# A retention layer and two expert layers in one kernel: decay tables made on TensorE, states as half blocks, first loads in another order

## The chip, the cores and the metric

One core of one Trainium2 chip runs the whole program. The metric is the device time of one execution in microseconds; the kernel before has a median of 1234.87 us over 3 runs (1234.5 to 1235.02).

## The reference

All arrays are float32. Retention is attention without a softmax: the score of query i and key j of head h is scaled and multiplied by gamma_h to the power i - j, and is zero for j > i. Two feed-forward layers follow on 4608 tokens of width 512.

```
gamma = 1.0 - 2.0 ** (-5.0 - arange(8))            # q, k, v: 8 x 8 heads x 576 x 64
ret = (q @ k.T / 8) * where(rel >= 0, gamma ** rel, 0)
x = ret @ v                                        # as 4608 x 512
h = max(x @ w1, x @ w2, x @ w3); x = h @ w_out     # 512 -> 768 -> 512
out = ((x @ u1) * (x @ u2)) @ u3 @ u_out           # 512 -> 1024 -> 1024 -> 512
```

## The kernel before, in words

**Two parts.** The first, 17 steps in the loop over m up to STEPS, computes the retention, two pairs of heads per step; there are 32 pairs n (a batch and two heads each). The second is a loop over 126 units of the dense products in four stages B, C, I, O. u3 and u_out follow each other with nothing between, so the first part also folds them into one matrix, in quarters of an eighth (wc_quarter). Every dense product is made from a high and a low fp32r part, so weights and tokens are split: ScalarE casts the high part, VectorE or GpSimd subtracts it for the low part.

**Retention in chunks.** A pair has 576 positions, which are 4 chunks of 128 and a tail of 64. Within a chunk TensorE makes scores (scores, L1000 and L1005), VectorE multiplies them by a table dec of powers of gamma (decay_scores L850, decay_tail L858), and TensorE multiplies by the values (values, L1048). Between chunks a state is carried: TensorE sums keys times decayed values (sum_state, L1021), VectorE scales the last state and adds (make_state, L872 and L875), and TensorE multiplies states by decayed queries (query_state, L1037). The two heads of a pair are 64 partitions each, so most matmuls use half of the array: rows or columns. query_state alone uses the whole array, on a 128 x 128 state with zeros outside the two diagonal blocks:

```
ps[:, bank, cols] += state[:, c - 1, :].T @ qdec[:, c - 1, :]
```

ScalarE decays the values (decay_values, L705, a factor per partition from vtab), reads results x (read_values, L716 and L721) and copies the folded block out (read_wc, L738); GpSimd decays the queries (decay_queries) with the table qtab. Where GpSimd works, the profile shows the helper's line, L589.

**What sets the order.** Each engine's program is written out by hand and waits on counting semaphores. Within step m TensorE makes the scores of pairs 2m and 2m + 1, then the quarters of that step, then query_state of the last step's pairs, sum_state of this step's, and values of the last step's. Quarters begin with step 3 (WC_FROM), two a step. The scores of pair n wait until x of pair n - 3 is read out (x_out), since they share a bank. All transfers are issued by SP in the order of its program: first the loads of pairs 0 to 3 with the tables between them, then step by step u3T and u_out blocks, keys for the next step, queries and keys (qk) for the step after it, stores of x, and values. The keys have two buffers; the queries four, the values six. A wait in SP's program holds all issues behind it.

## Time and profile before

| | |
|---|---|
| median of 3 runs | 1234.87 us |
| the profiled execution's own time | 1234.69 us |
| its span | 1232.9 us |
| TensorE matmul busy | 1216.6 us, 99% |
| VectorE, ScalarE, GpSimd busy | 761.3, 486.4, 433.7 us |
| transfers | 169.96 MB, mean 138 GB/s |

PE is TensorE (PEld its weight loads), DVE VectorE, ACT ScalarE, POOL GpSimd, SPq the issues of SP. A float32 matmul leaves two records. Times of a timeline count from the span's start. The first part ends near 177 us.

### The profile page before, as it was taken

Reading aid. Unit: us, or ns where it says so; the run is one execution under the profiler, and the core shown is the slowest. Engines: PE = TensorE matmul, PEld = TensorE weight load, DVE = VectorE, ACT = ScalarE, POOL = GpSimd, SP = SyncE. Lnnn points to the kernel's source line nnn. Section 1 sums busy time; section 2 is a strip of 40 time slices with the busy share of each in tenths; the row PEclk is TensorE's granted clock in tenths of the full one; section 3 lists DMA queues with packets and bytes.
Section 4 is the critical chain, followed back from the end, with each engine's and each line's share of the span. In section 5 each row is a group of like instructions: output and inputs, shape, how many; then the busy total and the mean of one; then the engine's idle time right before and its main releaser. Section 6 shows DMA issues by size and latency. Waiting matters only on the chain. (4 is left out here: it accounts for less than half of the span.)

```text
span 1232.9 us, 21160 instructions
## 1 busy us (share of the span) xinstructions
PE 1216.6 (99%) x8288; PEld 1202.2 (98%) x8288; DVE 761.3 (62%) x1192; ACT 486.4 (39%) x779; POOL 433.7 (35%) x234
## 2 busy tenths in 40 slices
PE   6999999999999999999999999999999999999999
PEld 5999999999999999999999999999999999999998
DVE  5666957844546364658876777453535366776553
ACT  3433544523223232326555544242323234554441
POOL 2644628220100102052967761202020217366550
PEclk9999999999999999999999999999999999999999
DMA  9999944120202112053455441213131343444441
GB/s 332 322 335 352 337 144 163 46 84 33 96 27 88 41 52 77 27 173 127 170 208 195 156 154 59 103 52 109 52 116 52 110 165 109 154 154 161 156 159 65
DMA packets 88084, 169.96 MB, mean 138 GB/s; under 512 B 9904, under 2 KB 59184, under 8 KB 87984
## 3 DMA queue, kind: packets, MB, share of 16 engines
q1 hardware_dynamic: 87984, 168.60, 39.3%
q8 instruction: 66, 1.08, 0.4%
q14 instruction: 34, 0.28, 0.1%
HBM read 106.70 MB, written 61.87 MB: 137 GB/s over the span
## 5 line engine op out<-in xcount | busy, mean ns | idle before, releaser
L1100 PE MATMUL ps<-chi,whi 128*128 128x384 f32 x2016 | 674.2, 334 | 2.1 <-ACT w L831 1.1
L1102 PE MATMUL ps<-chi,wlo 128*128 128x384 f32 x2016 | 673.5, 334 | 0.0
L1101 PE MATMUL ps<-clo,whi 128*128 128x384 f32 x2016 | 673.5, 334 | 0.0
L589 POOL TENSOR_TENSOR raw<-raw,raw 128x768 f32<-128x768 f32 (+3 forms) x102 | 267.1, 2640 | 588.8 <-DMA raw<-xd 203.6
L1100 PEld LDWEIGHTS ps<-chi,whi 128*128 128x128 f32 x2016 | 378.4, 188 | 4.2 <-ACT w L831 1.8
L1101 PEld LDWEIGHTS ps<-clo,whi 128*128 128x128 f32 x2016 | 378.5, 188 | 0.0
L1102 PEld LDWEIGHTS ps<-chi,wlo 128*128 128x128 f32 x2016 | 378.5, 188 | 0.0
L840 DVE TENSOR_TENSOR clo<-raw,chi 128x768 fp32r<-128x768 f32 (+2 forms) x168 | 252.4, 1530 | 31.8 <-ACT chi L763 31.8
L763 ACT CAST chi<-raw 128x768 fp32r<-128x768 f32 (+2 forms) x168 | 180.4, 1081 | 85.4 <-PE ps L1102 53.4
L831 ACT COPY w<-ps 128x384 f32<-128x384 f32 x126 | 60.6, 481 | 240.7 <-PE ps L1102 239.2
L818 ACT COPY u<-ps 128x384 f32<-128x384 f32 x126 | 60.7, 481 | 160.6 <-PE ps L1102 158.9
L956 DVE TENSOR_TENSOR h<-ps,u 128x384 f32<-128x384 f32 x66 | 36.6, 555 | 123.4 <-PE ps L1102 123.4
L930 DVE TENSOR_TENSOR h<-ps,w 128x384 f32<-128x384 f32 x66 | 36.6, 555 | 100.3 <-PE ps L1102 96.8
L930 DVE TENSOR_TENSOR w<-ps,w 128x384 f32<-128x384 f32 x60 | 33.4, 556 | 86.8 <-PE ps L1102 86.6
L797 ACT COPY s<-ps 128x384 f32<-128x384 f32 x126 | 60.5, 481 | 56.7 <-PE ps L1102 56.6
L810 ACT COPY h<-ps 128x384 f32<-128x384 f32 x66 | 31.6, 479 | 86.6 <-PE ps L1102 84.5
L956 DVE TENSOR_TENSOR u<-ps,u 128x384 f32<-128x384 f32 x60 | 33.2, 554 | 51.1 <-PE ps L1102 51.1
L840 DVE TENSOR_TENSOR wlo<-wraw,whi 128x768 fp32r<-128x768 f32 (+4 forms) x42 | 61.8, 1482 | 2.5 <-POOL wraw L589 2.3
L589 POOL TENSOR_TENSOR qdec<-qks,qtab 128x512 f32<-128x512 f32 x32 | 42.2, 1339 | 50.6 <-PE ps L1037 36.7
L589 POOL TENSOR_TENSOR wraw<-w,wraw 128x256 f32<-128x256 f32 (+2 forms) x21 | 24.7, 1177 | 92.2 <-DMA w<-wC 66.0
L589 POOL TENSOR_TENSOR wraw<-wraw 128x256 f32<-128x256 f32 (+2 forms) x42 | 47.4, 1130 | 1.6
L746 ACT CAST whi<-wraw 128x768 fp32r<-128x768 f32 (+4 forms) x42 | 43.9, 1054 | 5.0 <-POOL wraw L589 5.0
(43 smaller groups left out, 829.9 us busy)
## 6 DMA issues: line engine op xcount, KB each, us to landing
...
```

What stands on the lines that cost most here:

```text
L589: return nc.gpsimd.tensor_tensor(out_, a, b, op)
L746: nc.scalar.copy(whi[wi][:, s, :, :], wraw[wi][:, s, :, :]).then_inc(w_hi, 1)
L763: nc.scalar.copy(chi[st][pos][:, :, :], raw_block(tau, pos)[:, :, :]).then_inc(c_hi, 1)
L797: nc.scalar.copy(sbuf_s[it % 2][:, :], ps[:, X[it % 2], 0:N]).then_inc(s_made, 1)
L818: nc.scalar.copy(sbuf_u[it % 2][:, :], ps[:, X[it % 2], 0:N]).then_inc(u_made, 1)
L831: nc.scalar.copy(sbuf_w[it % 2][:, :], ps[:, X[it % 2], 0:N]).then_inc(w_made, 1)
L840: return nc.vector.tensor_tensor(out_, whole, hi.bitcast(f32), ALU.subtract)
L930: nc.vector.tensor_tensor(to[:, :], ps[:, Z[g % 2], 0:N], sbuf_w[g % 2][:, :], ALU.add).then_inc(sum22, 1)
L956: nc.vector.tensor_tensor(to[:, :], ps[:, Z[g % 2], 0:N], sbuf_u[g % 2][:, :], ALU.add).then_inc(sum12, 1)
L1100: nc.tensor.matmul(to, w1, x1, start=(start and k == 0), stop=False, skip_group_check=True)
L1101: nc.tensor.matmul(to, w1, x2, start=False, stop=False, skip_group_check=True)
L1102: last = nc.tensor.matmul(to, w2, x1, start=False, stop=(k == KH[st] - 1), skip_group_check=True)
```

## The change

Four things change.

1. The tables dec and qtab are no longer loaded. A small table of powers (pows, 8 partitions, one per head) is loaded, and TensorE makes the tables as outer products of powers by key and powers by query; VectorE masks the result to dec and ScalarE copies qtab. The value factors, a factor per partition for the states and the mask come in one other small load, cols. Fourteen matmuls on zeros (run_idle) stand between the first real ones.
2. A state is 128 x 64: each head has its block on its own partitions, and make_state works on both heads in one instruction with a factor per partition. query_state has two matmuls of 64 x 64 for each of before.
3. Loads: first keys and queries of pair 0 behind the two small tables; keys 0 to 3 have buffers of their own; the tails of the values are loaded apart, for two pairs at once, and so are the values from pair 4 on. Up to step 3 keys stand ahead of u3T and u_out. One of the u_out blocks is split on VectorE.
4. Quarters: step 3 has one of its two, step 4 has three, two of them at the step's end. Blocks of the stages C and O are loaded with a wait for each block.

```diff
 def quarters(m):
+    if m == WC_FROM:
+        return range(1)
+    if m == WC_FROM + 1:
+        return range(1, 2)
     if m >= STEPS - 2:
         return range(QUARTERS - 4 * (STEPS - m), QUARTERS - 4 * (STEPS - m) + 4)
     return range(2 * (m - WC_FROM), 2 * (m - WC_FROM) + 2) if m >= WC_FROM else ()
 
 
+def late_quarters(m):
+    return range(2, 4) if m == WC_FROM + 1 else ()
+
+
+
 
 U3_LOAD = {min(2 * kb + WC_FROM - 2, STEPS - 3): kb for kb in range(FT2)}
 U3_SPLIT = {min(2 * kb + WC_FROM - 1, STEPS - 2): kb for kb in range(FT2)}
-UO_LOAD = {1: (0, 1), 2: (2, 3)}
-UO_SPLIT = {2: (0, 1), 3: (2, 3)}
+UO_SPLIT = {2: (0,), 3: (1,), 4: (2, 3)}
...
+        dec = at("dec", [P, 2, 2, 2, CH], f32, o); o += HEADS * CH * 4
+        qtab = at("qtab", [P, PAIRS * CH], f32, o); o += PAIRS * CH * 4
+        cols = at("cols", [P, HEADS + PAIRS + CH], f32, o); o += (HEADS + PAIRS + CH + 4) * 4
+        vtab, gtab = cols[:, 0:HEADS], cols[:, HEADS:HEADS + PAIRS]
+        mask = cols[:, HEADS + PAIRS:]
+        pows = at("pows", [HEADS, 3 * P + PAIRS * CH], f32, 21504)
         vdec = [at(f"vdec{i}", [P, NC, P], f32, o + i * NC * P * 4) for i in range(2)]
...
+            def load_two_v(m):
+                n = 2 * m
                 if n >= 6:
-                    sp.wait_ge(valued, n - 5)
-                sp.dma_start(vs[n % 6][:, 0:NC * CH], vv[n, :, :]).then_inc(v_loaded[n % 6], 16)
-                sp.dma_start(vs[n % 6][TAIL:P, NC * CH:], vt[n, :, :]).then_inc(v_loaded[n % 6], 16)
+                    sp.wait_ge(valued, n - 4)
+                sp.dma_start(vs[:, n % 6:n % 6 + 2, 0:NC * CH], vv[n:n + 2, :, :].rearrange("n p c -> p n c")
+                             ).then_inc(v_loaded[v_sem(n)], 16)
+
+            def load_tails(m):
+                n = 2 * m
+                sp.dma_start(vs[TAIL:P, n % 6:n % 6 + 2, NC * CH:], vt[n:n + 2, :, :].rearrange("n p c -> p n c")
+                             ).then_inc(vt_loaded[m % 3], 16)
 
             def load_k(n):
-                if n >= 2:
+                if n >= 4:
                     sp.wait_ge(state_summed, n - 1)
-                sp.dma_start(ks[n % 2][:, :], kk[n, :, :]).then_inc(k_loaded[n % 2], 16)
+                sp.dma_start(keys_of(n)[:, :], kk[n, :, :]).then_inc(k_loaded[n % 4], 16)
...
-                for pos in (0, 3, 6, 2):
-                    if pos != 6 or t == 0 or st != O:
-                        load_raw_block(tau, pos)
-
-            def load_raw_rest(tau):
-                sp.wait_ge(c_lo, 7 * tau)
-                load_raw_block(tau, 6)
-
-            def load_decay(i, heads):
-                sp.dma_start(dec[:, heads, :], decay[:, heads, :]).then_inc(dec_loaded[i], 16)
-
+                for pos in blocks:
+                    if t and st in (C, O):
+                        if pos != 6 or st == O:
+                            sp.wait_ge(c_lo, 7 * (tau - 1) + pos + 1)
+                    load_raw_block(tau, pos)
+
+            sp.dma_start(pows[:, :], powers).then_inc(pows_loaded, 16)
+            sp.dma_start(cols[:, :], columns).then_inc(cols_loaded, 16)
             load_qk(0)
-            load_decay(0, slice(0, 2))
-            sp.dma_start(vtab[:, :], vdecay).then_inc(vtab_loaded, 16)
             load_v(0)
             load_k(0)
             load_qk(1)
-            load_decay(1, slice(2, 4))
             load_v(1)
             load_k(1)
             load_qk(2)
-            sp.dma_start(qtab[:, :, :], qdecay).then_inc(qtab_loaded, 16)
             load_qk(3)
-            load_decay(2, slice(4, HEADS))
             load_v(2)
             load_v(3)
+            load_k(2)
+            load_k(3)
+            load_tails(0)
             for m in range(STEPS):
+                if 0 < m < 4:
+                    for n in made_in(m + 1):
+                        load_k(n)
+                if m == 2:
+                    load_uo(1)
                 if m in U3_LOAD:
                     load_u3(U3_LOAD[m])
-                for i in UO_LOAD.get(m, ()):
-                    load_uo(i)
+                if m == 1:
+                    load_uo(0)
                 if m in P1_W_LOAD:
                     load_weight(P1_W_LOAD[m])
-                for n in made_in(m + 1):
-                    load_k(n)
+                if m >= 4:
+                    for n in made_in(m + 1):
+                        load_k(n)
                 for n in made_in(m + 2):
                     load_qk(n)
+                if m == 2:
+                    load_uo(2)
+                    load_uo(3)
                 for n in read_in(m):
                     if n >= PAIRS:
                         store_x(n)
-                for n in made_in(m + 2):
-                    load_v(n)
+                if m == 0:
+                    load_tails(1)
+                if 2 * m + 4 < NP:
+                    load_two_v(m + 2)
+                    load_tails(m + 2)
...
             for m in range(STEPS - 1):
+                for i in UO_SPLIT.get(m, ()) if m == 4 else ():
+                    split_uo(i)
                 if m in U3_SPLIT:
                     split_u3(U3_SPLIT[m])
-                for i in UO_SPLIT.get(m, ()):
-                    split_uo(i)
                 for n in made_in(m):
                     decay_queries(n)
+                for i in UO_SPLIT.get(m, ()) if m == 3 else ():
+                    split_uo(i)
...
-            for n in made_in(0):
-                decay_values(n)
+            act.wait_ge(idle_zeroed, 1)
+            nc.scalar.copy(idle[:, CH + 1:CH + 2], idle[:, CH:CH + 1])
+            decay_values(0)
+            act.wait_ge(qtab_powers, 1)
+            nc.scalar.copy(qtab[:, :], ps[:, S_WC, :]).then_inc(qtab_made, 1)
+            decay_values(1)
             for m in range(STEPS):
-                if m in U3_SPLIT:
+                if m == 2:
                     split_u3(U3_SPLIT[m])
                 for i in UO_SPLIT.get(m, ()):
                     split_uo(i)
+                if m in U3_SPLIT and m != 2:
+                    split_u3(U3_SPLIT[m])
                 if m in WC_READ:
                     read_wc(WC_READ[m])
                 for n in read_in(m):
...
             def make_state(n):
                 p = n % PAIRS
                 bank = S_WC if n == 1 else S_STATE
                 dve.wait_ge(state_summed, n + 2 - n % 2 if n >= 2 else n + 1)
                 for c in range(NC):
-                    for h in range(2):
-                        own = slice(h * DH, h * DH + DH)
-                        new = ps[own, bank, (n % 2 * NC + c) * DH:(n % 2 * NC + c + 1) * DH]
-                        if c == 0:
-                            nc.vector.tensor_copy(state[n % 2][own, c, own], new).then_inc(state_made, 1)
-                        else:
-                            dve.wait_ge(state_made, 2 * NC * n + 2 * (c - 1) + h + 1)
-                            nc.vector.scalar_tensor_tensor(
-                                state[n % 2][own, c, own], state[n % 2][own, c - 1, own], CHUNK_DECAY[2 * p + h], new,
-                                ALU.mult, ALU.add).then_inc(state_made, 1)
+                    new = ps[:, bank, (n % 2 * NC + c) * DH:(n % 2 * NC + c + 1) * DH]
+                    if c == 0:
+                        nc.vector.tensor_copy(state[n % 2][:, c, :], new).then_inc(state_made, 1)
+                    else:
+                        dve.wait_ge(state_made, NC * n + c)
+                        nc.vector.scalar_tensor_tensor(state[n % 2][:, c, :], state[n % 2][:, c - 1, :],
+                                                       gtab[:, p:p + 1], new, ALU.mult, ALU.add
+                                                       ).then_inc(state_made, 1)
+
+
+            def mask_decay(i):
+                if i == 0:
+                    dve.wait_ge(cols_loaded, 16)
+                dve.wait_ge(dec_powers, i + 1)
+                nc.vector.tensor_tensor(
+                    dec[:, i, :, :, :].rearrange("p h n c -> p (h n) c"),
+                    ps[:, 2 + i, :].rearrange("p (n c) -> p n c", c=CH),
+                    mask.unsqueeze(1).broadcast_to([P, 4, CH]), ALU.mult).then_inc(dec_made, 1)
+
+            def split_uo(i):
+                dve.wait_ge(uo_hi, i + 1)
+                low(uolo[:, 2 * i:2 * i + 2, :], uoraw[:, 2 * i:2 * i + 2, :], uohi[:, 2 * i:2 * i + 2, :]
+                    ).then_inc(uo_lo[i], 1)
...
+            nc.vector.memset(idle[:, :], 0.0).then_inc(idle_zeroed, 1)
             for i in range(4):
                 nc.vector.memset(probs[i][0:TAIL, :, NC * CH:SEQ], 0.0).then_inc(zeroed, 1)
-            for i in range(2):
-                nc.vector.memset(state[i][:, :, :], 0.0).then_inc(zeroed, 1)
             for i in range(6):
-                nc.vector.memset(vs[i][0:TAIL, NC * CH:], 0.0).then_inc(zeroed, 1)
-            dve.wait_ge(zeroed, 12)
+                nc.vector.memset(vs[0:TAIL, i, NC * CH:], 0.0).then_inc(zeroed, 1)
+            dve.wait_ge(zeroed, 10)
             for m in range(STEPS):
+                if m == 0:
+                    mask_decay(0)
                 for n in made_in(m):
                     decay_scores(n)
                     if n == 0:
+                        mask_decay(1)
                         make_state(n)
                 for n in made_in(m):
                     decay_tail(n)
...
                 for n in made_in(m):
                     if n:
                         make_state(n)
+                if m == 2:
+                    split_uo(0)
...
+                if n == 1:
+                    pe.wait_ge(dec_made, 2)
...
             def query_state(n):
-                pe.wait_ge(state_made, 2 * NC * (n + 1))
+                pe.wait_ge(state_made, NC * (n + 1))
                 pe.wait_ge(q_decayed, n + 1)
                 if n >= NP - 2:
                     pe.wait_ge(x_out, n - 1)
                 pe.wait_ge(decayed, min(3 * (n - n % 2 + 2) + 2 * (n % 2 + 1), 3 * NP))
                 for c in range(1, NC + 1):
                     bank, cols = x_cols(n, c)
-                    last = nc.tensor.matmul(ps[:, bank, cols], state[n % 2][:, c - 1, :],
-                                            qdec[n % 2][:, c - 1, 0:min(CH, SEQ - c * CH)],
-                                            start=(c == 1 or c == NC), stop=False, skip_group_check=True)
+                    for h in range(2):
+                        own = slice(h * DH, h * DH + DH)
+                        last = nc.tensor.matmul(ps[own, bank, cols], state[n % 2][own, c - 1, :],
+                                                qdec[n % 2][own, c - 1, 0:min(CH, SEQ - c * CH)],
+                                                start=(c == 1 or c == NC), stop=False, skip_group_check=True)
                 last.then_inc(queried, 1)
...
+            def run_idle(count, bank):
+                for _ in range(count):
+                    nc.tensor.matmul(ps[:, bank, 0:CH], idle[:, 0:CH], idle[:, 0:CH], start=True, stop=True,
+                                     skip_group_check=True)
+
+
+            def decay_powers(i):
+                for h in range(2):
+                    last = nc.tensor.matmul(ps[:, 2 + i, h * 2 * CH:(h + 1) * 2 * CH], pows[:, h * P:(h + 1) * P],
+                                            pows[:, 3 * P + i * 2 * CH:3 * P + (i + 1) * 2 * CH],
+                                            start=True, stop=True, skip_group_check=True)
+                last.then_inc(dec_powers, 1)
+
+            def query_powers():
+                nc.tensor.matmul(ps[:, S_WC, :], pows[:, 2 * P:3 * P], pows[:, 3 * P:], start=True, stop=True,
+                                 skip_group_check=True).then_inc(qtab_powers, 1)
+
+            pe.wait_ge(idle_zeroed, 1)
+            run_idle(5, S_STATE)
+            pe.wait_ge(pows_loaded, 16)
+            decay_powers(0)
+            pe.wait_ge(zeroed, 10)
             for m in range(STEPS):
                 for n in made_in(m):
                     scores(n)
-                    if m == 0:
-                        sum_state(n)
+                    if n == 0:
+                        decay_powers(1)
+                        query_powers()
+                        sum_state(0)
+                        pe.wait_ge(qtab_made, 1)
+                        run_idle(3, S_WC)
+                    if n == 1:
+                        pe.wait_ge(state_made, NC)
+                        run_idle(3, S_STATE)
+                        sum_state(1)
+                        run_idle(3, S_STATE)
                 for i in quarters(m):
                     wc_quarter(i)
                 for n in read_in(m):
                     sum_state(n)
                 for n in read_in(m):
                     values(n)
+                for i in late_quarters(m):
+                    wc_quarter(i)
...
+    by_query = np.zeros((HEADS, PAIRS, CH))
+    by_key = np.zeros((HEADS, 3, P))
+    for h in range(HEADS):
+        by_query[h, h // 2] = gamma[h] ** steps / np.sqrt(DH)
+        by_key[h, h % 2] = gamma[h] ** -steps
+        by_key[h, 2, h % 2 * DH:(h % 2 + 1) * DH] = 1.0
+    powers = np.concatenate([by_key.reshape(HEADS, -1), by_query.reshape(HEADS, -1)], axis=1)
+    vdecay = gamma[None, :] ** (CH - steps)[:, None]
+    chunk = np.repeat((gamma ** CH).reshape(PAIRS, 2).T, DH, axis=0)
+    columns = np.concatenate([vdecay, chunk, rel >= 0], axis=1)
     rows = lambda a: a.reshape(NP, 2, SEQ, DH).transpose(0, 1, 3, 2).reshape(NP, P, SEQ)
```

TensorE at the start. Before (qks are queries and keys, vdec decayed values):

```order
L1000 MATMUL ps<-qks_239 128x128 [waits qk_loaded0,zeroed]
L1000 MATMUL ps<-qks_239 128x128 x7
L1005 MATMUL ps<-qks_239 128x64 x2
L1021 MATMUL ps<-vdec_258,ks_249 64x64 [waits k_loaded0,v_decayed]
L1021 MATMUL ps<-vdec_258,ks_249 64x64 x7
L1000 MATMUL ps<-qks_240 128x128 [waits qk_loaded1]
```

The same place now:

```order
L1148 MATMUL ps<-idle 128x128 [waits idle_zeroed]
L1148 MATMUL ps<-idle 128x128 x4
L1154 MATMUL ps<-pows 128x256 [waits pows_loaded]
L1154 MATMUL ps<-pows 128x256
L1070 MATMUL ps<-qks_239 128x128 [waits qk_loaded0,zeroed]
...
L1154 MATMUL ps<-pows 128x256 x2
L1160 MATMUL ps<-pows 128x512
L1091 MATMUL ps<-vdec_256,ks_first_246 64x64 [waits k_loaded0,v_decayed]
...
L1148 MATMUL ps<-idle 128x128 [waits qtab_made]
L1148 MATMUL ps<-idle 128x128 x2
L1070 MATMUL ps<-qks_240 128x128 [waits dec_made,qk_loaded1]
```

Matmuls on zeros and on powers now stand ahead of the scores of pairs 0 and 1, and those of pair 1 also wait for the second half of dec and, through the idle ones, for qtab.

ScalarE in step 4. Before (wcst is the folded block, raw and xst hold x):

```order
L732 CAST u3hi_233<-u3raw_237 128x1024 [waits u3_loaded1]
L738 COPY wcst<-ps 128x512 [waits wc_done]
L716 COPY raw_6_55<-ps 128x192 [waits valued]
L721 COPY xst<-ps 128x384
```

The same place now, behind the decayed values of pairs 8 and 9:

```order
L771 CAST uohi<-uoraw 128x1024 [waits uo_loaded2]
L771 CAST uohi<-uoraw 128x1024 [waits uo_loaded3]
L777 CAST u3hi_233<-u3raw_237 128x1024 [waits u3_loaded1]
L783 COPY wcst<-ps 128x512 [waits wc_done]
L761 COPY raw_6_55<-ps 128x192 [waits valued]
L766 COPY xst<-ps 128x384
```

Two casts have moved from step 3 to here, and the copy of the folded block keeps its place although its quarter now is the last work of TensorE's step.

## Rows read from the trace of the kernel before

**Rows 1.** The page, busy time: engine, busy us (share of the span), instructions.
```profile
PE 1216.6 (99%) x8288; PEld 1202.2 (98%) x8288; DVE 761.3 (62%) x1192; ACT 486.4 (39%) x779; POOL 433.7 (35%) x234
```
**Rows 2.** TensorE's waits, whole span: engine, line, releaser: total, times, longest (us).
```profile
PE ps L1000 <- DMA qks<-qk: 6.0, 2, 4.4
PE ps L1037 <- DVE probs L850: 2.0, 2, 1.1
...
PE ps L1000 <- DVE probs L858: 1.0, 1, 1.0
```
**Rows 3.** TensorE's timeline, first scores of steps: start us, us, instructions, [idle before <-releaser].
```profile
4.42 2.08 PE L1000 MATMUL ps<-qks 64*128 64x128 f32 x16 [4.42 <-DMA qks<-qk]
...
10.36 2.08 PE L1000 MATMUL ps<-qks 64*128 64x128 f32 x16 [1.60 <-DMA qks<-qk]
...
14.77 1.16 PE L1000 MATMUL ps<-qks 64*128 64x128 f32 x16 [1.02 <-DVE probs L858]
...
23.35 1.16 PE L1000 MATMUL ps<-qks 64*128 64x128 f32 x16
...
33.58 1.16 PE L1000 MATMUL ps<-qks 64*128 64x128 f32 x16
...
53.82 1.16 PE L1000 MATMUL ps<-qks 64*128 64x128 f32 x16
```
**Rows 4.** TensorE's timeline within one later step.
```profile
69.18 1.90 PE L1037 MATMUL ps<-qdec,state 128*128 128x128 f32 x16
71.01 1.15 PE L1021 MATMUL ps<-vdec,ks 128*64 128x64 f32 x32
71.99 2.15 PE L1048 MATMUL ps<-probs,vs 128*64 128x128 f32 x40
74.07 1.16 PE L1000 MATMUL ps<-qks 64*128 64x128 f32 x16
75.07 0.34 PE L1005 MATMUL ps<-qks 64*128 64x64 f32 x4
75.24 1.11 PE L1000 MATMUL ps<-qks 64*128 64x128 f32 x16
76.18 0.34 PE L1005 MATMUL ps<-qks 64*128 64x64 f32 x4
76.45 0.50 PE L1063 MATMUL ps<-uohi,u3hi 128*128 128x512 f32 x1
```
**Rows 5.** All transfers, 0 to 20 us and 20 to 40 us.
```profile
DMA packets 2964, 6.23 MB, mean 311 GB/s; under 512 B 478, under 2 KB 990, under 8 KB 2963
...
DMA packets 2765, 7.23 MB, mean 361 GB/s; under 512 B 335, under 2 KB 591, under 8 KB 2762
```
**Rows 6.** An issue on SP (start, us); issues by line: count, KB, us to landing.
```profile
1.18 0.42 SPq L494 DMA_DIRECT2D dec<-decay  x1
...
vtab<-vdecay SPq DMA_DIRECT2D x1, 4.0 KB, 3.1
```
**Rows 7.** Groups of instructions, 0 to 60 us: busy us, mean ns | idle before, releasers.
```profile
L850 DVE TENSOR_TENSOR probs<-ps,dec 128x512 f32<-128x512 f32 x24 | 15.0, 683 | 5.8 <-PE ps L1005 5.6
...
L705 ACT ACTIVATE vdec<-vs,vtab 128x256 f32<-128x256 f32 x24 | 10.4, 504 | 10.2 <-DMA vs<-vt 10.2
L589 POOL TENSOR_TENSOR uolo<-uoraw,uohi 128x1024 fp32r<-128x1024 f32 x4 | 9.4, 2363 | 1.3 <-ACT uohi L726 1.3
...
L726 ACT CAST uohi<-uoraw 128x1024 fp32r<-128x1024 f32 x4 | 4.2, 1048 | 0.9 <-DMA uoraw<-uo 0.9
L716 ACT COPY raw<-ps 128x192 f32<-128x192 f32 (+1 forms) x12 | 4.1, 374 | 14.0 <-PE ps L1048 14.0
...
L858 DVE TENSOR_TENSOR probs<-ps,dec 64x128 f32<-64x128 f32 x12 | 3.0, 290 | 0.2
L721 ACT COPY xst<-ps 128x384 f32<-128x384 f32 x4 | 1.9, 485 | 0.0
...
L738 ACT COPY wcst<-ps 128x512 f32<-128x512 f32 x1 | 0.6, 585 | 2.1 <-PE ps L1067 2.1
```

93 lines of the change are left out of this document (49 added, 44 removed).

## The prediction

> **What bounds the kernel now.** I read the page's busy table first: TensorE works in 99% of the span [rows 1], so only three things can save time: idle time of TensorE, matmuls that run slowly, and matmuls that are fewer or shorter. The list of TensorE's waits comes next [rows 2]. Three of its entries make 9.0 us: 6.0 for the loads of queries and keys, 2.0 and 1.0 for the decayed scores. TensorE's timeline says where [rows 3]: all before step 3 at 33.58. From there a step takes (53.82 - 33.58) / 2 = 10.12 us and none of these waits is in it. The same rows show slow matmuls: 16 records of the scores take 2.08 us at 4.42 and at 10.36, and 1.16 at 14.77. The profile's granted clock reads 1.00, the 2.4 GHz level, throughout, so it does not print this; but a factor of 1.8 is what the 1.2 GHz level would do, and TensorE had idled 4.42 us before the first. I take it as that. Two scores and two state sums at half speed cost about 3.5 us.
>
> The detailed timeline of one full step gives its parts by differences of starts [rows 4]: queries times state 71.01 - 69.18 = 1.83; state sums 0.98; values 2.08; scores 76.45 - 74.07 = 2.38; the two folded quarters are the rest of 10.12, 2.85, so 1.4 each.
>
> The traffic of the transfers is the second limit at the start [rows 5]: 6.23 MB in the first 20 us and 7.23 in the next 20, so 0.36 MB per us with the engines always busy. A score load is 0.59 MB, a values or keys load 0.26, a load of u3T or uo 0.52.
>
> **The change, part by part.**
>
> *Queries times state (L1037), 64 x 64.* Two half matmuls on opposite quadrants take the place of each full one. The trace has no such pair. Its nearest rows are the values, where two column halves of one bank run side by side: 32 wide and 8 narrow records in 2.08 us, which is 16 wide pairs and 4 narrow ones, 18 units of 0.116. The new form has 24 wide and 8 narrow records per step, 14 units, 1.62 us: 0.21 less than 1.83. The change also puts a new switch of array shape behind the quarters. Scores to quarters, where the shape changes, takes 0.27 from start to start, and the first scores' tail to the next scores, where it does not, 0.17 [rows 4]: 0.10 for the switch. Net 0.11 a step. The bounds: side by side, as here, and one after the other, 3.23 us. I take the first, since both ways in which this kernel already halves the array run side by side.
>
> The Trainium skill, in TensorEngine Tiling (Array Packing), Restrictions and Gotchas, speaks against it: different row tiles can't access the same PSUM bank at the same time. The new halves are two row tiles that write one bank, in different partitions; the scores write different banks, and the values use no row tiles, so no row here shows the case. By that rule it would be 3.23 us a step; it is a rival below.
>
> *Tables from outer products.* Gone are 0.77 MB of tables, added about 0.1 MB. Queries and keys of pair 0 become the third issue of SP's queue. An issue takes 0.42 us [rows 6], so they land at 4.42 + 0.8 = 5.2. TensorE is not idle until then: five idle matmuls run from 1.2 on (0.46 each at the slow level, twice 1.83 / 8 of a matmul of L1037, its eight full ones taken alike [rows 4]), then the first powers, 2 x 256 columns, 1.8 us, which need a small table; one landed 3.1 us after its issue before [rows 6], so 3.2 to 5.0. All this is hidden. If the fast level is reached by 5.2, scores 0 end at 6.4 instead of 6.8. Behind them stand 2 x 256 and 512 columns more, 1.8 us at the fast level and on the path: 8.2. The state sum of pair 0 follows, 8.7. ScalarE copies the query table (0.6), TensorE waits for that and runs three idle matmuls, 9.7. Queries 1 have 1.8 MB ahead of their end instead of 1.9, without the small rows of the tables, and TensorE met them at 10.36 [rows 3]; I take 9. Scores 1 end at 10.9. VectorE decays them and the tails (2 x 0.68 and 2 x 0.29 [rows 7]), so scores 2 begin at 13.0 instead of 14.77. Idle matmuls and the state sum of pair 1 lie in that gap. The wait for VectorE before the queries stays. Step 1 then has 0.2 less in the queries and half of VectorE's state operations: scores 4 at 20.9 instead of 23.35. **Gain there 2.4.**
>
> *Steps 2 to 4, loads in another order.* Keys now come ahead of u3T and uo. In step 2 before, keys stood behind u3T and two blocks of uo, 1.6 MB or 4.3 us; now they have landed by 22 and are used at 25.6, so step 2 has only the wait for VectorE, and step 3 begins at 28.7 instead of 33.58. Adding loads in their new order at 0.36 MB per us from 6.23 MB at 20 us, queries and keys 6 and 7 are there by 28.3, just in time; 8 and 9 by 36; the rest of uo by 39; values 8 and 9 (13.7 MB) by 40.8, say 40, since 0.67 MB of table went. Step 3 now holds one quarter, 8.5 us: step 4 begins at 37.2.
>
> *Step 4 pays back.* It holds three quarters, two of them last. Their uo halves are cast by ScalarE behind the decayed values 8 and 9: 40 + 4 x 0.50 = 42, then 1.05 each, 44; GpSimd's two lows of 2.36 [rows 7] end at 47.7. TensorE is through its other work at 45.6 and quarter 2 at 47.0, so it waits 0.7 and ends at 49.1. And then a new wait: the copy of the folded block (L738) stands in ScalarE's queue ahead of the reads of x 6 and 7, and now waits for the end of quarter 3. Scores 10 wait for x 6: 0.59 + 0.37 + 0.49 [rows 7] and the ways between the engines, 1.8 us in all. Step 5 begins at 50.9 instead of 53.82. **Gain to here 2.9.**
>
> *Steps 5 to 16.* Twelve steps with 0.11 less: 1.3. VectorE loses half of its state operations, which ends no wait there. GpSimd, ScalarE and the transfers stay below TensorE. The loads of two values at once wait for the later pair, but the stores ahead of them in SP's queue wait for that too.
>
> *The later products.* The blocks of the second and fourth stage are loaded in finer steps. TensorE waited for none of them: nothing. If the new waits held a block back, the cost would be a fraction of a block's use, under 1 us.
>
> The sum: 2.9 + 1.3 = 4.2 against the profiled execution's own 1234.69, which lies 0.18 below the median of 1234.87. Forecast **1230.4 us**.
>
> **Rivals.**
> *A, slower: the two halves of L1037 don't run side by side.* Then 3.23 us a step instead of 1.62, 16 x 1.6 = 25.8 more: 1256. For it: that they share a bank as row tiles, which nothing in the trace does. Against: each half writes its own partitions, as in the values. The point from which it decides is 4.2 / 16 = 0.26 above 1.62: at 1.9 us a step the change is worth nothing. Chance 0.10.
> *B, no change: the start doesn't get earlier.* The fast level comes late (scores 0 end at 7.6 and the powers behind them take up to twice 1.8: 2 to 3 us), or values 8 and 9 land 1.5 us later and all of the late quarters with them. 2 to 3 us of the gain go: 1232.5 to 1234. For it: the chain has several links that are met by 0.5 us. Chance 0.18.
> *C, faster still: transfers are quicker than 0.36 MB per us,* since small packets of the tables are gone. Then the wait for uo in step 4 vanishes (0.7) and steps 2 and 3 begin up to 1.5 earlier; 1227.5 to 1228.5. Chance 0.17.
> *D, the new waits grow:* queries of steps 3 to 5, loaded later behind keys and uo, stall TensorE in each step by 1 to 2 us: 1235 to 1237. Against it: the sum of bytes has fallen. Chance 0.05.
> The forecast has 0.50.
>
> **How the numbers follow.** A measurement of this kernel tells 0.2%, 2.5 us, from no change. The forecast, C and a small part of B lie below 1232.4: faster 0.73. Most of B and half of D: same 0.15. A and the rest of D: slower 0.12. The range reaches from C's end with the rate still better, 1226.5, to the slow end of D, 1236; A and what is beyond the ends stay outside, about 0.15.
>
> **What would show it.** Right: 32 records of the new L1037 in about 1.6 us between quarters and state sums; scores 0 near 5.2 and in 1.2 us; scores 2 at 13, 4 at 21, 6 at 29; step 5 at 51; a wait of about 1.8 for ScalarE's read of x in front of scores 10; a step of 10.0 afterwards. Wrong: 3 us in that place (A); 16 score records still in 2.1 us at 5.2, or waits for queries in steps 3 to 5 (B, D).

## The result and the profile after

The changed kernel takes **1238.11 us** (median of 14 runs, 1237.08 to 1241.28), the kernel before 1234.95 beside it (14 runs, 1233.21 to 1237.62). The ratio is 1.0030, 95% interval 1.0022 to 1.0038: slower by 3.2 us, where 1230.4 was forecast, and outside the range given. The profiled execution took 1237.08 with a span of 1235.2.

The page, busy time, after, answering to [rows 1]:
```profile
PE 1226.3 (99%) x8582; PEld 1204.3 (97%) x8582; DVE 736.0 (60%) x1066; ACT 486.4 (39%) x781; POOL 434.1 (35%) x233
```
TensorE is busy for 10 us more than before, VectorE for 25 less. TensorE's waits, after, answering to [rows 2]:
```profile
PE ps L1136 <- POOL uolo L632: 1.4, 2, 0.7
PE ps L1070 <- ACT xst L766: 1.4, 1, 1.4
PE ps L1109 <- DVE probs L900: 1.1, 4, 0.4
```
The 6.0 us for queries and keys are gone, and the 3.0 for decayed scores have become 1.1. In their place are not only waits, but above all work: the timeline of TensorE after, from the start, then two rows of a later step, answering to [rows 3, 4]:
```profile
1.05 2.50 PE L1148 MATMUL ps<-idle 128*128 128x128 f32 x10 [1.05 <-DVE idle L955]
3.48 2.07 PE L1154 MATMUL ps<-pows 8*128 8x256 f32 x4
5.59 2.08 PE L1070 MATMUL ps<-qks 64*128 64x128 f32 x16
...
7.92 2.07 PE L1154 MATMUL ps<-pows 8*128 8x256 f32 x4
9.78 1.91 PE L1160 MATMUL ps<-pows 8*128 8x512 f32 x2
...
14.25 1.66 PE L1070 MATMUL ps<-qks 64*128 64x128 f32 x16
...
18.36 1.16 PE L1070 MATMUL ps<-qks 64*128 64x128 f32 x16
...
26.34 1.16 PE L1070 MATMUL ps<-qks 64*128 64x128 f32 x16
...
34.33 1.16 PE L1070 MATMUL ps<-qks 64*128 64x128 f32 x16
...
43.19 1.16 PE L1070 MATMUL ps<-qks 64*128 64x128 f32 x16
...
53.12 0.50 PE L1136 MATMUL ps<-uohi,u3hi 128*128 128x512 f32 x1 [0.73 <-POOL uolo L632]
...
55.46 0.50 PE L1136 MATMUL ps<-uohi,u3hi 128*128 128x512 f32 x1 [0.69 <-POOL uolo L632]
...
58.48 1.16 PE L1070 MATMUL ps<-qks 64*128 64x128 f32 x16 [1.37 <-ACT xst L766]
...
73.57 0.39 PE L1140 MATMUL ps<-uohi,u3lo 128*128 128x512 f32 x1
73.89 1.76 PE L1109 MATMUL ps<-qdec,state 64*64 64x128 f32 x32
75.57 1.15 PE L1091 MATMUL ps<-vdec,ks 128*64 128x64 f32 x32
```
Read it in three pieces. At the start, three groups of powers take 6.05 us together, the first scores 2.08 and the second 1.66, so TensorE is at its 1.2 GHz level until about 15.3 (an estimate: 1.66 lies between the 2.08 of the low level and the 1.16 of the high one, so the level changed within this group). The profile's granted clock does not show it: it reads 1.00 from the start on. Step 1 begins at 18.36 (before 14.77 [rows 3]). Steps 1 and 2 are then short, 7.98 and 7.99, so step 3 begins at 34.33, just 0.75 behind before. Step 4 has the three quarters and all new waits: 43.19 to 58.48, 4.66 behind before's 53.82. Later, the queries on halves take 75.57 - 73.89 = 1.68, and a full step 10.08 (68.56 to 78.64).

All transfers after, 0 to 20 us and 20 to 40 us, answering to [rows 5]:
```profile
DMA packets 2474, 5.94 MB, mean 297 GB/s; under 512 B 275, under 2 KB 643, under 8 KB 2473
...
DMA packets 2308, 5.77 MB, mean 288 GB/s; under 512 B 226, under 2 KB 498, under 8 KB 2305
```
Before it was 6.23 and 7.23 MB. The bytes of the second 20 us are not needed less, they come later. SyncE's issues after show where:
```profile
17.79 0.97 SPq L437 DMA_DIRECT2D vs<-vt  x1
24.00 0.82 SPq L443 DMA_DIRECT2D ks<-kk  x2
24.86 0.43 SPq L462 DMA_DIRECT2D u3raw<-u3T  x1
```
For 5.2 us SyncE issues nothing. Keys 4 (L443) wait for the state sum that frees their buffer (`sp.wait_ge(state_summed, n - 1)`), and u3T and uo, whose buffers are free, stand behind them in the one queue. The same stretch by windows (PE, PEld, DVE, ACT, POOL busy, PEclk, DMA share, GB/s):
```profile
20.00:24.00 4.00, 3.43 (x72) 3.14 (x70) 2.72 (x6) 0.00 (x0) 1.70 (x2) 1.00 0.39 135
```
ScalarE's timeline after, in step 4, then GpSimd's, tells what the lateness becomes:
```profile
47.97 1.71 ACT L750 ACTIVATE vdec<-vs,cols 128x256 f32<-128x256 f32 x4 [3.96 <-DMA vs<-vv]
49.58 1.98 ACT L771 CAST uohi<-uoraw 128x1024 fp32r<-128x1024 f32 x2
...
57.15 0.58 ACT L783 COPY wcst<-ps 128x512 f32<-128x512 f32 x1 [4.65 <-PE ps L1140]
```
```profile
50.68 4.72 POOL L632 TENSOR_TENSOR uolo<-uoraw,uohi 128x1024 fp32r<-128x1024 f32 x2 [6.26 <-ACT uohi L771]
```
Values 8 and 9 land at 47.97, the casts of uo stand behind them, GpSimd's lows behind those, and quarters 2 and 3 on TensorE wait 0.73 and 0.69. The copy of the folded block at 57.15 then holds the reads of x, and scores 10 wait 1.37.

From step 5 to the products the change takes 181.49 - 58.48 = 123.01, before 177.47 - 53.82 = 123.65. The products take 1053.7 against 1055.4. So in the profiles what was lost was lost by step 5, and some of it came back in the products, for which nothing had been forecast.

### The profile page after: what moved, and what is told of

The parts are those of the page before. It is cut to its first block, busy times and chain, and to the rows that moved or that the text cites. A ratio compares the mean times of both kernels' runs of the same rounds, so it can differ in the third digit from the quotient of the medians.

```text
span 1235.2 us, 21640 instructions
## 1 busy us (share of the span) xinstructions
PE 1226.3 (99%) x8582; PEld 1204.3 (97%) x8582; DVE 736.0 (60%) x1066; ACT 486.4 (39%) x781; POOL 434.1 (35%) x233
## 4 chain that ended last, share of the span: by engine, by line
PE 96%; DMA 2%; DVE 1%; issue 1%; ACT 0%; POOL 0%; SPq 0%; ACTq 0%; DVEq 0%; POOLq 0%
PE ps L1206 28%; PE ps L1208 28%; PE ps L1207 28%; PE ps L1070 2%; PE ps L1121 2%; PE ps L1109 2%; PE ps L1136 1%; PE ps L1091 1%; PE ps L1140 1%; PE ps L1138 1%; DMA vs<-vv 1%; DMA hd<-h 1%; PE ps L1148 0%; PE ps L1075 0%; POOL uolo L632 0%
## 5 line engine op out<-in xcount | busy, mean ns | idle before, releaser
L632 POOL TENSOR_TENSOR raw<-raw,raw 128x768 f32<-128x768 f32 (+3 forms) x102 | 270.5, 2673 | 579.2 <-DMA raw<-xd 202.5
L632 POOL TENSOR_TENSOR wraw<-w,wraw 128x256 f32<-128x256 f32 (+2 forms) x21 | 27.4, 1303 | 94.3 <-DMA w<-wC 66.7
L891 DVE TENSOR_TENSOR wlo<-wraw,whi 128x768 fp32r<-128x768 f32 (+4 forms) x42 | 57.8, 1387 | 2.8 <-POOL wraw L632 2.7
L900 DVE TENSOR_TENSOR probs<-ps,dec 128x512 f32<-128x512 f32 x64 | 39.8, 683 | 23.3 <-PE ps L1075 23.3
```

The costliest lines, as they stand in the source:

```text
L632: return nc.gpsimd.tensor_tensor(out_, a, b, op)
L891: return nc.vector.tensor_tensor(out_, whole, hi.bitcast(f32), ALU.subtract)
L900: nc.vector.tensor_tensor(probs[n % 4][:, h, 0:NC * CH].rearrange("p (n c) -> p n c", c=CH), ps[:, 2 * (n % 2) + h, :].rearrange("p (n c) ...
```

## The experiments

Theory W (warm-up): the start is late because the powers, matmuls on 8 rows, don't bring TensorE to the 2.4 GHz level. Theory Q (queue): the rest comes from the order of the loads and the late quarters. Rivals: the idle matmuls do the harm by their zeros or their length; the halves cost what the rule on banks says. Each result has its own runs of the kernel before beside it (medians 1234.52, 1234.36, 1234.57 and 1234.86 for the four batches). Diffs are against the changed kernel unless it is said otherwise.

### More idle matmuls, of zeros and of a constant

zeros40:
```diff
-            run_idle(5, S_STATE)
+            run_idle(40, S_STATE)
```
const40 has the same, and
```diff
-            nc.vector.memset(idle[:, :], 0.0).then_inc(idle_zeroed, 1)
+            nc.vector.memset(idle[:, :], 0.3).then_inc(idle_zeroed, 1)
```


> The change with 40 instead of 5 matmuls on zeros at the start; the whole later program is only pushed back. In the profile of the change an idle matmul took 0.48 us (two records) from 1.05 us on, and the fast level was there only at about 15.3 us. Theory Z (matmuls on zeros do not bring the fast level): all 40 take 0.46 to 0.50 us, 19 us in all, and the first scores after them still take 2.1 us for 16 records. Theory A (the level rises with time alone, about 15 us after the start): the matmuls after 15 us take 0.23 us whatever they work on. Theory B (a longer unbroken run is enough): the matmuls get short well before 15 us, after some 4 to 8 us.

> The same 40 matmuls on the constant 0.3 instead of zeros. If operands of zero were what kept the slow level (theory Z), these get short (0.23 us each) after some 4 to 8 us, where those on zeros do not. If data does not matter, both kernels switch at the same time.

One run each: 1246.69 and 1244.74 us, both longer by the idle matmuls. Timeline of TensorE in zeros40, then its windows (TensorE alone: busy, PEclk, DMA share, GB/s):
```profile
1.05 11.28 PE L1148 MATMUL ps<-idle 128*128 128x128 f32 x80 [1.05 <-DVE idle L955]
12.26 1.13 PE L1154 MATMUL ps<-pows 8*128 8x256 f32 x4
...
19.87 2.08 PE L1070 MATMUL ps<-qks 64*128 64x128 f32 x16
```
```profile
12.00:16.00 4.00, 4.00 (x32) 0.96 0.84 310
16.00:20.00 4.00, 4.00 (x26) 0.50 0.01 3
20.00:24.00 4.00, 4.00 (x43) 0.69 0.67 192
```
Behind 80 idle records the powers take 1.13 instead of 2.07, so the level was there. Then it is lost: a granted clock of 0.50 from 16 to 20, with TensorE busy all the time, behind the powers. The next scores take 2.08 again. const40 has the same windows (0.98, 0.50, 0.67) and 80 records in 11.36 us. So the values of the idle matmuls play no part, and something in the real work behind them lets the level fall. The windows from 0 to 8 read 1.00 here too, though only 14 records stand between 1.05 and 4 us, where 38 stand in 8 to 12: in these traces the granted clock does not show the low level at the start.

### What holds the level: matmuls on 8 rows, on 64, and on quadrants

probe_rows8 puts a prologue ahead of the work: 20 matmuls on the whole array, 60 on 8 rows, 20 whole ones. probe_halves has 20 whole, 80 on alternating 64 rows, 20 whole, 80 on alternating 64x64 quadrants.
```diff
-            run_idle(5, S_STATE)
+            probe(20, 128, 128, False)
+            probe(60, 8, 128, False)
+            probe(20, 128, 128, False)
```


> The change with a longer prologue in place of its five idle matmuls: 20 on the whole array (128 rows), 60 that use 8 rows as the powers do, 20 on the whole array again, all 128 columns wide and on zeros; the rest is pushed back. In the runs with 40 whole ones the fast level came after some 5 us and was lost again at about 15 us, behind the powers and the first scores. Theory P (a matmul on 8 rows does not count as activity): the first 20 end at the fast level, the 60 start at 0.23 us each and fall to 0.46 within some us (granted clock 0.50), and the last 20 bring the fast level back. Rival (the loss came from waits or from loads between the matmuls): the 60 stay at 0.23 us.

> The same with 20 whole ones, 80 on 64 rows by turns on either half (the form of the scores), 20 whole ones, 80 on 64 x 64 quadrants by turns (the form of the new queries times states). Theory P extended (activity goes by the part of the array in use): the level holds in the scores' form, two halves side by side being a whole array, and may fall in the quadrants' form, which uses half of it. Rival: both hold, and the falls of the level in the kernels come from waits alone.

One run each, 1267.46 and 1261.23 us, which counts nothing here. Windows of probe_rows8, then of probe_halves (columns as above, with all engines):
```profile
8.00:12.00 4.00, 4.00 (x38) 4.00 (x37) 0.00 (x0) 0.00 (x0) 0.00 (x0) 0.99 1.02 404
12.00:16.00 4.00, 4.00 (x21) 4.00 (x20) 0.00 (x0) 0.00 (x0) 0.00 (x0) 0.50 0.85 316
...
36.00:40.00 4.00, 4.00 (x38) 3.39 (x38) 1.01 (x2) 0.00 (x0) 0.00 (x0) 1.00 0.02 4
```
```profile
10.00:16.00 6.00, 6.00 (x112) 6.00 (x110) 0.00 (x0) 0.00 (x0) 0.00 (x0) 1.00 0.91 350
...
22.00:28.00 6.00, 6.00 (x111) 6.00 (x112) 0.00 (x0) 0.00 (x0) 0.00 (x0) 1.00 0.01 3
```
The 8-row matmuls stand from about 7 to 30 us. The clock reads 0.50 from 12 on, though TensorE is 100% busy; 21 records fit in 4 us instead of 38. The whole matmuls behind them bring it back by 36. Matmuls on 64 rows and on quadrants hold 1.00 throughout, and two of them run side by side: 112 records in 6 us, where whole ones make 38 in 4. So W's mechanism exists: a busy TensorE is not enough, if its matmuls use 8 rows. But the kernel has far fewer than 60 of them in a row, and its real work behind the two prologues gives a divided answer. Behind probe_rows8 the level falls again (0.50 from 44 to 46), as in zeros40. Behind probe_halves the same powers on 8 rows run fast and the level holds, with the clock at 1.00 in all windows to 60 us:
```profile
34.16 1.02 PE L1160 MATMUL ps<-pows 8*128 8x512 f32 x2
...
36.71 1.16 PE L1070 MATMUL ps<-qks 64*128 64x128 f32 x16
```
That the powers alone make the level fall is therefore not shown: in three of four kernels with a long prologue it fell behind them, in one it did not.

### The powers on all rows

padded keeps the powers but lays them in 128 rows, of which 120 are zero. The products are the same. It has 12 idle matmuls, and queries and keys 0 are loaded first:
```diff
-        pows = at("pows", [HEADS, 3 * P + PAIRS * CH], f32, 21504)
+        pows = at("pows", [P, 3 * P + PAIRS * CH], f32, 21504)
...
-            sp.dma_start(pows[:, :], powers).then_inc(pows_loaded, 16)
-            sp.dma_start(cols[:, :], columns).then_inc(cols_loaded, 16)
             load_qk(0)
+            sp.wait_ge(pows_zeroed, 1)
+            sp.dma_start(pows[0:HEADS, :], powers).then_inc(pows_loaded, 16)
+            sp.dma_start(cols[:, :], columns).then_inc(cols_loaded, 16)
...
+            nc.vector.memset(pows[:, :], 0.0).then_inc(pows_zeroed, 1)
...
-            run_idle(5, S_STATE)
+            run_idle(12, S_STATE)
```


> The change with 12 instead of 5 idle matmuls at the start, and the powers on all 128 rows (120 of them zeros) instead of 8; queries and keys of pair 0 are the first load. Theory clock (activity by rows used): the fast level comes at 5 to 7 us and holds, the powers behind the first scores take 2.0 us instead of 4.0, step 1 begins at 13 to 14.5 us instead of 18.36, and the total falls by 3 to 4 us. Rival (the level has other reasons): step 1 stays at 18 us or later, and the total rises with the longer prologue.

1235.59 us (1233.74 to 1238.02, 10 runs), ratio 1.0008 (0.9998 to 1.0018). Timeline of TensorE in padded:
```profile
5.57 1.03 PE L1157 MATMUL ps<-pows 128*128 128x256 f32 x4
6.53 1.16 PE L1073 MATMUL ps<-qks 64*128 64x128 f32 x16
...
14.93 1.16 PE L1073 MATMUL ps<-qks 64*128 64x128 f32 x16
...
30.90 1.16 PE L1073 MATMUL ps<-qks 64*128 64x128 f32 x16
...
53.94 1.16 PE L1073 MATMUL ps<-qks 64*128 64x128 f32 x16 [1.37 <-ACT xst L768]
```
The three groups of powers take 1.03, 1.13 and 1.02, the scores 1.16; step 1 begins at 14.93 and step 3 at 30.90, 3.4 us earlier than in the change. So the low level is what made the start late, worth 2 to 3 us of the time. What keeps it away is less clear, since the kernel differs from the change in three things. zeros40 had the longer idle stretch without the padding and lost the level behind the powers, which speaks for the rows; 12 idle matmuls with the powers on 8 rows were not run. And the kernel only draws level with before: its step 5 begins at 53.94, where before's is at 53.82, though its step 3 leads before's by 2.7. That loss is Q's.

### No idle matmuls; tables loaded again

no_idle takes out all the idle matmuls (`run_idle(5, S_STATE)` and the three groups of 3). loaded_tables takes out the powers as well and loads the decay tables as before:
```diff
             load_qk(0)
+            sp.dma_start(cols[:, :], columns).then_inc(cols_loaded, 16)
+            load_decay(0)
...
-            run_idle(5, S_STATE)
-            pe.wait_ge(pows_loaded, 16)
-            decay_powers(0)
...
-                        decay_powers(1)
-                        query_powers()
```


> The change without any of its 14 matmuls on zeros (the waits for the query table stay). If they help to reach the fast level, it comes later than 15.3 us and the second pair's scores start no earlier. If they do not help, the three ahead of the scores of pair 1 (1.65 us at the slow level in the profile of the change) and the six after them (1.9 us, partly in the wait for VectorE) go from the path: step 1 begins 2 to 3 us before 18.36, and 1 to 2.5 us of the total go, unless the late landing of pair 1's loads takes their place.

> The change with the two tables loaded as before (keys and queries of pair 0 first, then columns, half of dec, and so on) and no matmul on powers or zeros; all else stays as in the change: order of keys, half states, late quarters. Theory start (6.05 us of powers at the slow level, 4.0 of them behind the first scores): step 1 begins at 14 to 15.5 us instead of 18.36, and the total falls by 3 us or more, since step 5 follows it. Rival transfers (the loads are what counts; keys ahead of u3T and u_out leave the transfers idle): step 1 comes earlier but step 5 keeps its 58.5 within 1 us and the total falls by less than 1.

no_idle: 1238.82 us (1238.35 to 1241.62, 5 runs), 1.0035 (1.0022 to 1.0048), no different from the change. The idle matmuls neither harm nor help as they stand. In its profile step 1 begins earlier (17.15), but the level is lost again from about 37 to 42 (granted clock 0.50), behind waits of 0.82 and 1.57 us at 34.00 and 36.90.

loaded_tables: 1236.67 us (1233.52 to 1240.66, 10 runs), 1.0017 (1.0003 to 1.0032). Step 1 begins at 13.81, sooner than in any kernel with powers on 8 rows, yet step 3 only at 34.98 and step 5 at 56.80, with the same 1.37 of ScalarE. Two things lie between. Without any powers the level is low here for even longer:
```profile
13.81 2.08 PE L1059 MATMUL ps<-qks 64*128 64x128 f32 x16 [0.97 <-DVE probs L912]
```
and step 1 takes 23.79 - 13.81 = 9.98 us instead of 7.98. So powers on 8 rows are not the only start at which the high level comes late. Then TensorE stands still for 2.78 us within the values of step 2, with no releaser named. The late half of the loss remains without outer products. The time lies 1.4 us under the change, between the under 1 of one theory and the 3 or more of the other. The runs scatter by 7 us, and with the clock: the four longest (1239.06 to 1240.66) have a mean granted clock of 0.997 to 0.999, the six others (1233.52 to 1237.09) one of 1.000.

### Warm-up alone, halves alone, on the kernel before

warm_before adds 12 idle matmuls to the kernel before. halves_only gives it the 128x64 states with the factor per partition and the half matmuls, and nothing else. Against before:
```diff
+            for _ in range(12):
+                nc.tensor.matmul(ps[:, S_STATE, 0:CH], idle[:, 0:CH], idle[:, 0:CH], start=True, stop=True,
+                                 skip_group_check=True)
```
```diff
-                            nc.vector.scalar_tensor_tensor(
-                                state[n % 2][own, c, own], state[n % 2][own, c - 1, own], CHUNK_DECAY[2 * p + h], new,
-                                ALU.mult, ALU.add).then_inc(state_made, 1)
+                        nc.vector.scalar_tensor_tensor(state[n % 2][:, c, :], state[n % 2][:, c - 1, :],
+                                                       gtab[:, p:p + 1], new, ALU.mult, ALU.add
+                                                       ).then_inc(state_made, 1)
...
-                    last = nc.tensor.matmul(ps[:, bank, cols], state[n % 2][:, c - 1, :],
-                                            qdec[n % 2][:, c - 1, 0:min(CH, SEQ - c * CH)],
-                                            start=(c == 1 or c == NC), stop=False, skip_group_check=True)
+                    for h in range(2):
+                        own = slice(h * DH, h * DH + DH)
+                        last = nc.tensor.matmul(ps[own, bank, cols], state[n % 2][own, c - 1, :],
+                                                qdec[n % 2][own, c - 1, 0:min(CH, SEQ - c * CH)],
+                                                start=(c == 1 or c == NC), stop=False, skip_group_check=True)
```


> The kernel before with 12 matmuls on zeros, whole array, ahead of its first scores, and nothing else. With the powers on all rows these 12 brought the fast level at about 5 us. Expected: they end at 5.7 us instead of leaving TensorE free at 4.4, so the first scores start 1.2 us later but take 1.2 instead of 2.1; scores of pair 1 still wait for their load at 10.4 and take 1.2 instead of 2.3; step 1 begins 1 us before 14.77; total 0 to 1 us less. If the level falls again in the waits (0.8 and 3 us, no work on TensorE), the second scores still take 2.1 us and nothing is gained.

> The kernel before with the states as 128 x 64 alone (a factor per partition, two 64 x 64 matmuls for each full one); tables, loads and quarters as before. By the profile of the change the 32 records take 1.69 us between quarters and state sums instead of 1.83, and 0.10 of that goes to the switch in front. Expected: 10.08 us a full step instead of 10.12, 0.5 to 1 us less in all, within what a measurement tells. Rival (64 x 64 counts as less activity): the granted clock falls in some executions in steps 1 and 2, where there are no quarters, and the runs scatter upwards by 1 to 4 us.

warm_before: 1234.46 us (11 runs), 0.9994 (0.9985 to 1.0002). Both first scores run in 1.18 and 1.16, step 1 begins at 13.10 and step 5 at 52.40, 1.4 us before [rows 3], and the median shows 0.1 of that. Its first scores had to stand behind the idle matmuls until 6.47, and it still waits 1.24 and 0.60 us for queries. In its profile the lead is gone again in the products: they take 1057.2 us, before's 1055.4.

halves_only: 1233.86 us (11 runs), 0.9992 (0.9983 to 1.0000), 0.7 us faster at the edge of what can be told; its step is 10.07. The halves are worth about what 16 steps of 0.05 give.

### The later half: keys back, copy later

keys_back puts the loads of keys in steps 1 to 3 behind u3T and uo, as before:
```diff
-                if 0 < m < 4:
-                    for n in made_in(m + 1):
-                        load_k(n)
...
-                if m >= 4:
+                if m >= 1:
```
padded_wc is padded, with the folded block copied behind the reads of x in step 4; padded_wc_keys is padded_wc with the edit of keys_back:
```diff
-                if m in WC_READ:
+                if m in WC_READ and m != 4:
                     read_wc(WC_READ[m])
...
+                if m == 4:
+                    read_wc(0)
```


> The change with the keys of steps 1 to 3 back behind u3T and u_out in SP's program. In the change SP waits from 18.8 to 24.0 us for the state sum of pair 2 with u3T, u_out and the queries of step 3 queued behind, and the transfers stand still from 22 to 24.5 us. Theory transfers: without it the values 8 and 9 land 2 to 3 us before 47.97, the two waits for GpSimd's low parts in step 4 (1.4 us) go, step 5 begins 1 to 2.5 us before 58.5. Rival: the keys themselves are then late in step 2 (as before the change, 1 us) and gain nothing.

> The change with the powers on all rows and 12 idle matmuls (as in the run before), and in step 4 ScalarE reads x of pairs 6 and 7 before it copies the folded block. Theory late quarter: the wait of 1.4 us in front of scores 10 goes, step 5 begins 1.4 to 1.6 us before 53.94, total 1234.0 to 1234.3. Rival: the copy then comes later and quarter 4 waits for it instead, gain under 0.5.

> The same with the keys of steps 1 to 3 back behind u3T and u_out. If loads still bind in steps 3 and 4 (0.3 us of waits for the low part of u_out in the padded run), 0.3 to 0.8 us less than the run beside it; if the keys come too late for step 2 instead, 0.5 us or more above it.

keys_back: 1237.60 us, 1.0027 (1.0014 to 1.0039). One of its 7 executions took 1730 us at a mean granted clock of 0.656; it is not in the ratio, and the median of the six others is 1237.00. The two waits for uolo are gone from its profile, step 5 begins at 56.51 instead of 58.48, and the 1.37 of ScalarE stays; the median shows 1.1 of these 2.0 (0.4 by the ratios).

padded_wc: 1234.80 us (11 runs), 0.9998 (0.9989 to 1.0007), 0.8 less than padded by medians, with no wait for ScalarE in front of scores 10. Step 5 does not begin 1.4 earlier in its profile, as expected, but at 54.26: that execution waits 0.73 and 0.68 for uolo again, and 0.53 for queries. padded_wc_keys: 1232.22 us (12 runs), 0.9981 (0.9973 to 0.9990), another 2.6 less. So what the two edits undo costs about 3 us once the start is mended, most of it by the order of keys, u3T and uo. The profiles of both fell on long executions (1238.5 and 1236.14), with a wait of 2.2 us that only zeros40 has besides; from the waits of padded_wc_keys:
```profile
PE ps L1208 <- DVE wlo L892: 2.2, 1, 2.2
```
It stands in the products, in kernels that are the same there. It also fits the 2 us between zeros40 and const40. Why some executions have it, the runs don't tell.

### Folding as before, and with the powers padded

Both causes were still only bounded, so the later half was undone as a whole: old_fold has before's table of quarters (two in step 3, two in step 4), before's loads of uo, u3T and keys, and its casts. old_fold_padded adds the edit of padded.
```diff
 def quarters(m):
-    if m == WC_FROM:
-        return range(1)
-    if m == WC_FROM + 1:
-        return range(1, 2)
...
-    return range(2, 4) if m == WC_FROM + 1 else ()
+    return ()
...
-UO_SPLIT = {2: (0,), 3: (1,), 4: (2, 3)}
+UO_LOAD = {1: (0, 1), 2: (2, 3)}
+UO_SPLIT = {2: (0, 1), 3: (2, 3)}
```


> The change with the folding of u3 and u_out wholly as before: two quarters in each of steps 3 and 4 ahead of the queries, u3T and u_out loaded ahead of the keys, all low parts of u_out on GpSimd. Tables from powers on 8 rows, first loads and half states as in the change. Theory two causes (the start costs some 3 us at the slow level, the late quarters of step 4 some 3 us more): step 1 stays at 18.4, but step 5 begins near 55.5 instead of 58.48, and the total falls by 2 to 3 us, to 1235.0 to 1236.0. Rival one cause (the start alone): step 5 stays within 1 us of 58.5 and the total at 1238.

> The same with 12 idle matmuls at the start and the powers on all 128 rows. If the two causes add, step 1 begins at 15 to 16, step 5 at 52 to 53, and the total is 2.5 us under the run beside it, 1232 to 1233. If a load then binds in steps 2 and 3 (the kernel before had waits for keys and for queries there), under 1.5 us of it arrive.

old_fold: 1234.96 us (1234.02 to 1237.98, 11 runs), 0.9999 (0.9991 to 1.0008). old_fold_padded: **1231.85 us** (1230.54 to 1232.49, 6 runs), 0.9968 (0.9955 to 0.9981). A window of old_fold, the stretch in which the change has the hole, then the timeline of TensorE in old_fold_padded:
```profile
20.00:24.00 4.00, 3.43 (x64) 3.14 (x62) 2.98 (x6) 0.00 (x0) 1.26 (x2) 1.00 0.95 305
```
```profile
15.04 1.16 PE L1058 MATMUL ps<-qks 64*128 64x128 f32 x16
...
31.02 1.16 PE L1058 MATMUL ps<-qks 64*128 64x128 f32 x16
...
51.18 1.16 PE L1058 MATMUL ps<-qks 64*128 64x128 f32 x16
```
Here u3T is issued at 18.99 and uo at 19.62, ahead of keys 4 at 24.45, and the share of the transfers from 20 to 24 is 0.95 instead of 0.39. TensorE's busy time there is the same 3.43: the hole itself costs nothing where it stands, it is paid in step 4. From the change to old_fold the ratio falls from 1.0030 to 0.9999 and the median by 3.2 us; from there the three edits of padded bring 3.1 more (1234.96 to 1231.85). The two causes add, to about 1 us. old_fold_padded beats both kernels: 3.0 us below before, 6.3 below the change.

### The finer loads of the products alone

blocks_only gives the kernel before nothing but the change's finer loads of blocks in the second and fourth stages. Against before:
```diff
-                    sp.wait_ge(c_lo, 7 * (tau - 1) + 4)
-                for pos in (0, 3, 6, 2):
-                    if pos != 6 or t == 0 or st != O:
-                        load_raw_block(tau, pos)
+                for pos in blocks:
+                    if t and st in (C, O):
+                        if pos != 6 or st == O:
+                            sp.wait_ge(c_lo, 7 * (tau - 1) + pos + 1)
+                    load_raw_block(tau, pos)
```


> The kernel before with the loads of the blocks in stages C and O as in the change, nothing else. The products took 1055.4 us in the profile of before and 1053.7 in that of the change. Theory: the finer waits end the waits of 0.4 to 0.7 us at the starts of the stages and the total falls by 1 to 1.5 us. Rival: these waits move from run to run (other runs here had products of 1054 to 1058 us with the same blocks), and the total stays within 0.5 us of before.

1232.50 us (1230.78 to 1235.87, 11 runs), 0.9981 (0.9971 to 0.9990): 2.4 us faster. Waits of TensorE in the products, of the kernel before, then of blocks_only:
```profile
PE ps L1100 <- ACT w L831: 1.1, 2, 0.7
...
PE ps L1100 <- DVE h L930: 0.6, 1, 0.6
PE ps L1100 <- DVE clo L840: 0.4, 1, 0.4
```
```profile
PE ps L1101 <- ACT w L832: 0.6, 1, 0.6
```
In these two profiles 2.1 us of waits become 0.6, and the products take 1053.8 instead of 1055.4. That the finer loads make the kernel 2.4 us faster is shown by the times. That they do it by ending these waits is not: the waits move from execution to execution, as the rival had it. With the finer loads the products take 1053.5 to 1059.4 in 14 profiles (old_fold_padded has 2.7 us of such waits), without them 1055.4, 1057.0 and 1057.2 in three. The waits name ScalarE and VectorE, yet only loads were changed, so loads come late behind at least some of them.

## Why the prediction was wrong

By its own steps:

- **The fast level by 5.2, the powers at 1.8 us: this step failed.** It said "If the fast level is reached by 5.2" and then took it as reached. TensorE was indeed occupied from 1.05 on, but by five whole matmuls and then by powers on 8 rows, and the level came only near 15.3. The powers behind the first scores took 3.7 from start to start (7.92 to 11.62) instead of 1.8, the scores 2.08 and 1.66, and step 1 came at 18.36 instead of 13.0. These 5.4 us divide so. Scores 0 begin at 5.59 and not at 5.2: 0.4. From there to step 1 the change takes 12.77, and padded, at the fast level from its first powers on, 8.40 for the same instructions: 4.4 is the clock. The forecast had 7.8 for this stretch, so 0.6 is the chain itself, drawn too short. padded does not get back all of the 4.4, since its scores 0 stand behind a longer prologue until 6.53: it gains 3.4 at step 1 and 3.1 in the medians (old_fold against old_fold_padded). Rival B named the effect ("the fast level comes late") but priced it at 2 to 3 us. That a few matmuls on zeros and powers on 8 rows would not do for the high level is what the text had no rows for.
- **The loads at 0.36 MB per us "with the engines always busy": this step failed too.** It added bytes and forgot that a queue waits in order. Keys 4 in front of u3T and uo were said to have "landed by 22"; they could not be issued before 24.00, for lack of a free buffer, and held everything behind them. 5.77 MB moved from 20 to 40 us and not 7.2; values 8 and 9 came at 47.97 and not at 40. Some of that is the late start: padded has them at 43.38. Price: 3.2 us by medians, 3.8 by the ratios (change against old_fold). This is for the order of loads and the late quarters together; no run takes back the late quarters alone.
- **Step 4 pays back: right in kind.** The two waits in it were forecast as 0.7 for GpSimd and 1.8 for the read of x; they are 0.73 and 0.69, and 1.37. Forecast with them was a step of 13.7; it took 15.29, and 13.93 in padded.
- **The halves: right.** 1.68 us against 1.62 forecast and 3.23 for rival A. The switch is 73.89 - 73.57 = 0.32 from the last matmul of a quarter to the halves, where a quarter's own stand 0.23 apart: 0.09 against 0.10. A step is 0.04 shorter instead of 0.11: the old queries had taken 1.83, so 0.15 less the switch. Steps 5 to 16 and the rest of the first part took 0.64 less (123.01 against 123.65), where 1.3 was forecast. The Trainium skill, TensorEngine Tiling (Array Packing), Restrictions and Gotchas, says that row tiles can't access the same bank simultaneously; the 32 records in 1.68 us, two row tiles writing different partitions of one bank, don't bear it out.
- **"The later products: nothing": wrong by 2.4 us,** to the other side. It said that TensorE waited for none of the blocks. Four waits of less than a us each were in the profile, and none names a transfer; blocks_only shows that the loads had a price all the same.
- **Two slips that changed nothing.** The "about 3.5 us" for two scores and two state sums at half speed is 2.9 by the timeline of before (scores 2.39 against 1.33 twice, sums 1.12 and 1.06 against 0.69), and is no term of the sum. D ends at 1237 in its own text and at 1236 in the range.
- **Rival D** (1235 to 1237) came nearest in time, and not by its mechanism: no query stalled in steps 3 to 5. The slower side was to be reached by a late start and a late step 4 together, each of which stood in the text alone and at half its size.

The account: blocks -2.4, halves -0.7, start +3.1, loads and late quarters +3.2, which is +3.2 of 3.2 measured. That it comes out so exactly is luck, as each term is known to about 1 us. The start and the folding are priced with each other mended or not (padded alone gives 2.7 by its ratio to the change, 1.0008 against 1.0030), and agree to about 1 us. With both mended nothing of a gain by the outer products is left: old_fold_padded's -3.0 is what blocks and halves give alone (-3.1). The tables computed on the chip save 0.7 MB, and no run shows a us for it.

Open is what makes some executions of these kernels 3 to 5 us longer: a fall of the level in the waits of the first 45 us (seen in no_idle), the wait for wlo, or more. Open is also which of padded's edits brought the level, and when it comes at all: to the kernel before by 14.77 in its profile, and only at about 19 in those of halves_only and loaded_tables, none of which has powers. And a lead in the first part is not all kept: padded begins its products 4.5 us before the change (176.97 against 181.49) and takes 1.2 more in them.
